# A plain first product, by token halves, in the first supertile of a fused attention and two-layer kernel

## The reference

```python
scores = matmul(q_c, k_c.T) / 8            # 576 chunks of 64 tokens, 64 dims (batch 8, heads 8, 9 chunks)
attn = exp(scores - max); attn /= sum(attn) + 1e-9
x = matmul(attn, v_c)                      # to [4608 tokens, 512]
h = x @ w_in;  g = max(h, 0) + alpha * min(h, 0);  y = g @ w_out      # 512 -> 2048 -> 512
h = y @ w_in2; g = h - tanh(h);                    out = g @ w_out2
```

## Time and profile before

| | us |
|---|---|
| median of 3 runs | 1644.78 (1644.63 to 1649.84) |
| the profiled execution | 1645.04 |
| its span, first to last instruction | 1643.2 |
| TensorE busy | 1584.7 (96% of the span) |
| VectorE, ScalarE, GpSimd busy | 977.2, 671.3, 328.6 |
| first product of supertile 0 begins | 41.28 |
| first product of supertile 1 begins | 206.87 |

### The profile page before, as it was taken

How to read it: one execution, slowest core, us unless ns; L and a number is a source line. 1 busy time by engine, 2 the same in 40 slices (tenths; PEclk the granted TensorE clock), 3 DMA queues, 4 the chain that set the end, 5 groups by cost and what they waited for, 6 DMA issues and landing times.

```text
span 1643.2 us, 26691 instructions
## 1 busy us (share of the span) xinstructions
PE 1584.7 (96%) x10512; PEld 1487.1 (90%) x10512; DVE 977.2 (59%) x1351; ACT 671.3 (41%) x995; POOL 328.6 (20%) x454
## 2 busy tenths in 40 slices
PE   4879999999999999999999999999999999999999
PEld 3878899989999999999989988988988988988987
DVE  5557868766785776676674562562662562562542
ACT  4566535535553554554553241242232232232221
POOL 3684556676564200000000000000000000000000
PEclk9999999999999999999999999999999999999999
DMA  5477688769879756755734843853853843843842
GB/s 206 170 280 251 232 311 339 263 238 363 277 251 333 285 181 215 269 175 183 298 140 152 311 178 129 330 181 127 334 180 124 334 178 125 335 175 127 295 178 76
DMA packets 72938, 375.04 MB, mean 228 GB/s; under 512 B 9072, under 2 KB 13168, under 8 KB 38256
## 3 DMA queue, kind: packets, MB, share of 16 engines
q1 hardware_dynamic: 63216, 341.87, 57.7%
q0 software_dynamic: 9600, 31.46, 5.2%
HBM read 308.29 MB, written 65.01 MB: 227 GB/s over the span
## 4 chain that ended last, share of the span: by engine, by line
PE 86%; DVE 4%; DMA 3%; POOL 3%; issue 2%; ACT 2%; SPq 0%; ACTq 0%; POOLq 0%; DVEq 0%
PE banks L522 13%; PE banks L523 13%; PE banks L524 13%; PE banks L551 7%; PE banks L553 7%; PE banks L552 7%; PE banks L585 5%; PE banks L586 5%; PE banks L584 5%; PE a_bank L584 3%; PE a_bank L585 3%; PE a_bank L586 3%; DMA raw<-in_weights 2%; POOL ring L339 1%; DVE go_lo L960 1%
## 5 line engine op out<-in xcount | busy, mean ns | idle before, releaser
L522 PE MATMUL banks<-xo_hi,ring 128*128 128x384 f32 x1344 | 453.4, 337 | 20.1 <-POOL ring L339 7.6
L524 PE MATMUL banks<-xo_hi,ring 128*128 128x384 f32 x1344 | 452.2, 336 | 0.0
L523 PE MATMUL banks<-xo_lo,ring 128*128 128x384 f32 x1344 | 452.1, 336 | 0.0
L960 DVE TENSOR_TENSOR go_lo<-g_full,go_hi 128x768 fp32r<-128x768 f32 x288 | 287.1, 999 | 252.1 <-ACT go_hi L746 251.4
L746 ACT CAST go_hi<-g_full 128x768 fp32r<-128x768 f32 x288 | 239.6, 837 | 366.3 <-PE banks L586 223.5
L551 PE MATMUL banks<-go_hi,ring 128*128 128x384 f32 x768 | 265.6, 346 | 13.9 <-DVE go_lo L960 8.7
L522 PEld LDWEIGHTS banks<-xo_hi,ring 128*128 128x128 f32 x1344 | 254.6, 189 | 24.7 <-POOL ring L339 14.4
L553 PE MATMUL banks<-go_hi,ring 128*128 128x384 f32 x768 | 257.0, 335 | 0.0
L552 PE MATMUL banks<-go_lo,ring 128*128 128x384 f32 x768 | 256.8, 334 | 0.0
L523 PEld LDWEIGHTS banks<-xo_lo,ring 128*128 128x128 f32 x1344 | 254.6, 189 | 0.4
L524 PEld LDWEIGHTS banks<-xo_hi,ring 128*128 128x128 f32 x1344 | 254.5, 189 | 0.0
(11 more groups left out here) (98 smaller groups left out, 1924.1 us busy)
## 6 DMA issues: line engine op xcount, KB each, us to landing
ring<-w_split SPq DMA_DIRECT2D x242, 1024.0 KB, 5.5
qkv<-in_chunks SPq DMA_DIRECT2D x60, 384.0 KB, 5.0
w_split<-ring SPq DMA_DIRECT2D x22, 1024.0 KB, 5.1
w_split<-made_first POOLq DMA_DIRECT2D x44, 256.0 KB, 5.8
w_split<-sums POOLq DMA_DIRECT2D x44, 256.0 KB, 5.6
y_between<-stage SPq DMA_DIRECT2D x12, 768.0 KB, 7.2
x_raw<-y_between SPq DMA_DIRECT2D x6, 1536.0 KB, 9.4
out<-x_raw SPq DMA_DIRECT2D x36, 256.0 KB, 6.6
```

The lines of the kernel that those rows point to most:

```text
L522: nc.tensor.matmul(h, hi, xo_hi[:, o, k, :], start=fresh and k == 0, stop=False, skip_group_check=not fresh)
L523: nc.tensor.matmul(h, hi, xo_lo[:, o, k, :], start=False, stop=False, skip_group_check=not fresh)
L524: last = nc.tensor.matmul(h, lo, xo_hi[:, o, k, :], start=False, stop=k == 1, skip_group_check=not fresh)
L960: nc.vector.tensor_tensor(go_lo[:, slot, :, :], g_of(n), go_hi[:, slot, :, :], ALU.subtract).then_inc(glo_ready, 1)
```

## The change

Only stage 0 changes in what it computes; the other stages find the same blocks in `w_dram`.

- Phase A of stage 0 becomes a plain product with 8 blocks a pair in place of 7: the first 32 token-half t = 0 with all of the weights (`first_product(0, m)`, m = 0 to 15, two blocks each), then t = 1 with the same 32 blocks. Four operands of the input are split (B11, B21, B12, B22), no sums.
- The 32 blocks are made as before (cast, low part), stored one by one (`store_block`, 256 KB), those of A21 to a new `w_a21`, and loaded again for the second half (`load_blocks`, groups 8 to 15).
- `first_product(0, 0)` to `(0, 4)` lie between the attention units 3 to 5 of supertile 0, whose `probs` get two more buffers.
- ScalarE reads each bank with two Relus (`act_first`), VectorE finishes it (`activate_first`).
- GpSimd makes the 32 sum blocks (S1 to S4 of 8 pairs), which stage 1 on need, with `keep_block`: 8 of them after the last of the 32 low parts, the other 24 each after one low part of the second product's blocks. It reloads raw weights for that into one buffer, `raw[:, 0]` (`load_again`); the raw weights of the second product share `raw[:, 1]`.
- Stage 0 has 96 blocks (`FIRST_BLOCKS`); block 64 + n is that of unit n. SP's `load_unit` calls stand after `store_block` of units 0, 1, 15, 19, 23 and 28.

```diff
+FIRST_BLOCKS, SLICES = 96, 32
+FIRST_GROUPS = FIRST_BLOCKS // PER_GROUP
...
+            def load_again(p):
+
+                for i in range(2):
+                    nc.gpsimd.dma_start(raw[:, 0, i, :], weights[p + PAIRS * i, :, 0:DM]).then_inc(raw_again_in, 16)
...
+            def keep_sum(layer, p, i, step, k):
...
+                if i:
+                    pool.wait_ge(made_step, step)
+                    pool.wait_ge(made_low, k)
+                if i == 0:
+                    nc.gpsimd.tensor_tensor(s3, a11, a21, ALU.subtract).then_inc(made_step, 1)
+                elif i == 1:
+                    nc.gpsimd.tensor_tensor(a21, a21, a22, ALU.add).then_inc(made_step, 1)
+                elif i == 2:
+                    nc.gpsimd.tensor_tensor(s2, a21, a11, ALU.subtract).then_inc(made_step, 1)
+                else:
+                    nc.gpsimd.tensor_tensor(s2, a12, s2, ALU.subtract).then_inc(made_step, 1)
+                pool.wait_ge(made_step, step + 1)
+                keep_block(layer, product_at(layer, (7, 5, 6, 3)[i], p), k, (s3, a21, s2, s2)[i])
+
+            def sum_of_first(k):
+
+                p, i = divmod(k, 4)
+                if i == 0:
+                    pool.wait_ge(raw_again_in, 32 * (p + 1))
+                keep_sum(0, p, i, k, k)
+                if i == 3 and p + 1 < PAIRS:
+                    pool.wait_ge(made_low, k + 1)
+                    load_again(p + 1)
...
-            for j in range(BLOCKS):
-                what, i, p = block_use(0, j)
-                if what == "product" and i == (6 if p else 1):
-                    weight_sums(0, j, p)
-                low_part(0, j)
-            pool.wait_ge(wlo_ready, BLOCKS)
+            for j in range(SLICES):
+                low_part(j)
+            pool.wait_ge(wlo_ready, SLICES)
+            load_again(0)
+            for k in range(8):
+                sum_of_first(k)
+            for n in range(units_in(0)):
+                low_part(2 * SLICES + n)
+                if n < 24:
+                    sum_of_first(8 + n)
...
+            def first_product(t, m):
...
+                for half in range(2):
+                    j = SLICES * t + 2 * m + half
+                    o = (B12, B22)[half] if t else (B11, B21)[half]
+                    weights_ready(0, j)
+                    if m == 0:
+                        pe.wait_ge(xlo_ready, x_count(0, o))
+                    w = block_of(0, j)
+                    for k in range(2):
+                        hi, lo = w[:, 0, k * P:(k + 1) * P], w[:, 1, k * P:(k + 1) * P]
+                        nc.tensor.matmul(h, hi, xo_hi[:, o, k, :], start=half == 0 and k == 0, stop=False)
+                        nc.tensor.matmul(h, hi, xo_lo[:, o, k, :], start=False, stop=False)
+                        last = nc.tensor.matmul(h, lo, xo_hi[:, o, k, :], start=False, stop=half == 1 and k == 1)
+                    last.then_inc(block_done, 1)
...
+            scores(5)
+            first_product(0, 0)
+            output(3)
+            first_product(0, 1)
+            transpose_attn(4)
+            first_product(0, 2)
+            output(4)
+            first_product(0, 3)
+            transpose_attn(5)
+            first_product(0, 4)
+            output(5)
+            for m in range(5, 16):
+                first_product(0, m)
+            for m in range(16):
+                first_product(1, m)
+            phase_b(0)
...
+            def act_first(t, m):
...
+                nc.scalar.activation(g_full[:, p, 2 * half + t, :], h, ACT.Relu)
+                nc.scalar.activation(part[:, m % 4, :], h, ACT.Relu, scale=-1.0).then_inc(h_read, 1)
...
+            for m in range(4, 16):
+                high_parts(2 * m + AHEAD)
+                act_first(0, m)
+            for m in range(16):
+                high_parts(SLICES + 2 * m + AHEAD)
+                act_first(1, m)
...
+                nc.vector.scalar_tensor_tensor(mine, part[:, m % 4, :], minus_alpha[:, f:f + 1], mine,
+                                               ALU.mult, ALU.add).then_inc(g_ready, 1)
...
+            def first_supertile():
+                for j in range(SLICES):
+                    if j >= 3 and j % 4 == 3 and j // 4 + 2 < PAIRS:
+                        load_raw(j // 4 + 2)
+                    store_block(j)
+                load_raw_second(0)
+                load_raw_second(1)
+                for group in range(8, 16):
+                    load_blocks(group)
+                for n in range(units_in(0)):
+                    if n % 2 == 1 and n // 2 + 2 < 16:
+                        load_raw_second(n // 2 + 2)
+                    store_block(2 * SLICES + n)
+                    if n in (0, 1, 15, 19, 23, 28):
+                        load_unit(UPS + (0, 1, 15, 19, 23, 28).index(n))
+                store_y(0, 0)
+                for group in range(FIRST_GROUPS, FIRST_GROUPS + RING - 1):
+                    load_group(group)
```

More of the change, by code:

```diff
@@ L77, in units_in, with unit_at @@
     return 32 if layer == 0 else 16
[L80 to L82 removed]
+def unit_at(s, n):
+    if s == 0:
+        return 2 * SLICES + n
+    if layer_of(s) == 0:
         return 55 if n == 0 else 56 + n
@@ L89, in unit_slice, with pairs_by @@
     return n % 16 // 2 + PAIRS * (n % 2)
[L92 to L116, removed]
+def pairs_by(q):
+    return sum(1 for p in range(PAIRS) if min(product_at(0, i, p) for i in range(1, 8)) < PER_GROUP * (q + 1))
 def fused_kernel(nc, chunks, weights, alpha, out):
@@ L318, in _, with low_part @@
         def _(pool):
[L319 to L339, removed]
+            def low_part(j):
+                here = block_of(0, j)
+                pool.wait_ge(whi_ready, split_index(j) + 1)
+                nc.gpsimd.tensor_tensor(here[:, 1, :], raw_of(j), here[:, 0, :], ALU.subtract).then_inc(wlo_ready, 1)
+            def load_again(p):
+                for i in range(2):
+                    nc.gpsimd.dma_start(raw[:, 0, i, :], weights[p + PAIRS * i, :, 0:DM]).then_inc(raw_again_in, 16)
             def load_raw2(c):
@@ L616, in phase_b @@
             def phase_b(s):
-                if layer_of(s) == 0:
+                if s == 0:
+                    second_product(s, 0)
+                    for n in range(1, units_in(0)):
+                        attention(s, n)
+                        second_product(s, n)
+                elif layer_of(s) == 0:
                     second_product(s, 0, (0,))
@@ L647, in _ @@
         def _(act):
-            made = {s: 0 for s in range(RUNS) if made_here(s)}
-            def high_part(s, j):
-                layer = layer_of(s)
-                what, i, p = block_use(layer, j)
-                if j % PER_GROUP == 0 and s * GROUPS + j // PER_GROUP >= RING:
-                    before, last = group_last(s, j)
-                    act.wait_ge(block_done, done(before, last))
-                    if made_here(before):
-                        act.wait_ge(w_stored[(s * GROUPS + j // PER_GROUP) % RING], 16 * stores_of(before, last))
-                if what == "product" and i in (3, 5, 6, 7):
-                    act.wait_ge(w_sum, 4 * (layer * PAIRS + p) + {7: 1, 5: 2, 6: 3, 3: 4}[i])
-                else:
-                    c = raw_chunk(layer, j)
-                    act.wait_ge(raw_in[c % 2], 32 * raw_loads(layer, c))
-                nc.scalar.copy(block_of(s, j)[:, 0, :], raw_of(layer, j)).then_inc(whi_ready, 1)
@@ L1052, in _ @@
             shift(0)
-            for u in range(UPS):
-                if u + 1 < UPS:
-                    shift(u + 1)
-                normalize(u)
+            shift(1)
+            normalize(0)
+            shift(2)
+            normalize(1)
+            shift(3)
+            normalize(2)
+            shift(4)
+            normalize(3)
             low_x(0, B11)
@@ L1192, in _ @@
             for i in range(RING):
-                sp.wait_ge(w_stored[i], 16 * sum(1 for g in range(i, GROUPS * RUNS, RING) if made_here(g // GROUPS)))
+                sp.wait_ge(w_stored[i], 16 * stores_of(FIRST_GROUPS - RING + i))
 def kernel(q, k, v, moe_w_in, moe_w_out, moe_alpha, moe2_w_in, moe2_w_out):
```

467 lines of the change are left out of this document (270 added, 197 removed).

## The result

The changed kernel takes 1722.81 us (median of 4, 1720.43 to 1724.37); its ratio to the kernel before, run beside it (median 1645.99 of 4), is 1.0462, 95% interval 1.0439 to 1.0484. The forecast was 1721 in a range of 1690 to 1754. The profiled execution has a span of 1720.9 us, 77.7 more than before.

What follows compares the result with a forecast made beforehand. GpSimd was taken to bound the opening supertile: unit 23's low part at 240 plus 43 gives 283 against 206.9, 76 us lost on about 1645. Forecast 1721 us, range 1690 to 1754.

Steps and rivals of the forecast that it cites:

- The bound: Stage 0, second phase: GpSimd's low parts, queued behind its sums, decide when the second product can go on.
- First product: Opening of stage 0: begins near 36, first_product 5 near 55, other 27 calls at 2.08 us end near 111.
- TensorE still waits in the first product, for raw DMA: Rival, first product: the change does not do what it says; moves little, since GpSimd sets the end; no separate chance.
- Last low part: GpSimd, first half: the last of 32 low parts at 69 us (64 to 73).
- The ninth sum: GpSimd behind 69: three reload gaps (21.9) and 8 sums x 3.7 (29.6) put it at 120.5 (101 to 132).
- The cadence: GpSimd, second phase: four units take 21.45 us (18.5 to 26.8), from sums, low parts and a reload gap.
- T: End of unit 23's low part on GpSimd in the second phase: 240 us (204.5 to 281).
- T + 43: End of supertile 0, with attention loads in SP's queue holding TensorE at units 9, 14, 17, 21.
- T + 24: End of supertile 0 without the hold by attention loads: 1702 us; rival's chance 0.2, including quick sums with the hold.
- Behind it both programs are the same on TensorE: Behind the first product of supertile 1 (206.87 before): same distance to the end as before.
- GpSimd keeps up: Rival, loop over n: sum and low part fit TensorE's 2.6 us a unit; 1634 us; chance 0.04.
- The heavy case: Second phase: every GpSimd step behind a go_lo difference slow from port sharing, four units nearer 26.8 us, time near 1748.

Runs made afterwards that it cites:

- e_tworaw: Changed kernel with a second buffer for GpSimd's reload of raw weights for the sums, first pair loaded ahead of low part 24: 1697.57 us.
- e_both: Changed kernel with attention loads 8 to 11 behind stores of units 11, 15, 19, 23 and ScalarE casting 3 blocks ahead, not 10: 1718.72 us.
- e_free: e_both with the loads of attention units 8 to 11 moved to behind the stores of units 7, 11, 15, 20: 1702.86 us.
- e_behind: Changed kernel with the last 24 of the 32 weight sums made behind all low parts of the second product: 1698.04 us.
- e_best: Changed kernel with VectorE's old order, ScalarE casting 3 ahead, earlier attention loads, two reload buffers and GpSimd's sums spread: 1656.98 us, ratio to before 1.0057.

## Why the prediction was right, and where that was luck

**The bound.** GpSimd's low parts behind its sums set the end of stage 0. Right; shown by e_tworaw, which touched GpSimd alone in stage 0.

**First product.** Its end was put at 111 and is at 111.5. But two errors cancel: first_product(0, 5) began at 44.1, not 55 (the start at 29.6 and not 36, no long slow phase), and the 27 calls behind it took 2.50 us each, not 2.08, with 8.1 us of waits (5.2 of them for ScalarE's Relu, which stood behind casts that waited 3.7 and 3.0 us for raw chunks) and a granted clock of 0.93 from 36 to 60 us. Its rival "TensorE still waits in the first product, for raw DMA" came true in this form, and moved little, as it said. Last low part: 67.0 for 69.

**The ninth sum**: 115.1 for 120.5. Eight sums took 3.4 us each, with store waits of 2.8 and 0.35 us only, and not 3.7; the three gaps, from the end of the step before the load's issue, took 6.7, 8.2 and 5.7 us, for 7.3.

**The cadence**: 21.0 us for four units against 21.45. Gaps ran from 4.3 (ahead of 134.00) to 7.5 us (ahead of 219.90) around the 6.1 taken. DMA moved 159 to 211 GB/s in the four windows, not 145. T: 230.7 for 240, most of it from the ninth sum.

**Who holds TensorE behind T** is the step that failed: "T + 43" from SP's queue alone, with "T + 24" if that hold did not exist. It came to T + 50, and removing the hold alone gave T + 52. The signs named for it failed too: no wait for L339's low parts (here L344), and 7.4 us of waits for attention loads in all. What the prediction left out is ScalarE: it was said to have room in the first product, by the sum of its durations, and got no term in the second, while its list stands 10 blocks ahead at a raw buffer that GpSimd frees. It hides SP's queue, and SP's queue hides it; only without both does stage 1 follow at T + 28. The size was not bad: with ScalarE out of the way the hold cost 17 us of stage 1's start, 11 of them behind T (e_both against e_free), where the prediction had 19. The 9 us by which T came early and the 7 us by which the rest came late cancel too, so that 1721 is within 2 us of the measured time is luck; that it lies in the range is owed to GpSimd's cadence.

**Not seen**: low_g(2) ahead of activate_c11, 0.68 us in each of six stages, 4.1 us. "Behind it both programs are the same on TensorE" was true of TensorE's list, not of whom it waits for.

**Rivals.** "GpSimd keeps up" would have needed 2.6 us for a sum and a low part; the quickest sum was 2.9.

Contention: GpSimd's two-input operations take 0.72 to 0.76 us or up to 1.6, and the timelines show when. From 110 to 231 us after there are 71 of them. 21 overlap in time a VectorE operation with both inputs in SBUF, and 10 of these took 0.91 to 1.47 us; the 50 others all took 0.72 to 0.75. Before, from 60 to 200 us, 36 of 92 overlap one, 25 of them took 0.90 to 1.56 us, and none of the 56 others more than 0.76. Two meetings, one begun by VectorE and one by GpSimd (a go_lo difference that meets nothing takes 0.95 us):

```profile
197.04 0.95 DVE L1085 TENSOR_TENSOR go_lo<-g_full,go_hi 128x768 fp32r<-128x768 f32 x1
...
197.20 1.38 POOL L364 TENSOR_TENSOR made_first<-sums,made_first 128x256 fp32r<-128x256 f32 x1
...
221.18 0.74 POOL L364 TENSOR_TENSOR made_first<-sums,made_first 128x256 fp32r<-128x256 f32 x1
...
221.29 1.44 DVE L1085 TENSOR_TENSOR go_lo<-g_full,go_hi 128x768 fp32r<-128x768 f32 x1
```

This agrees with what the Trainium skill says in "SBUF — State Buffer", section "SBUF: two separate sides", of taking turns for a whole instruction. The heavy case did not come because few steps met: VectorE was busy 2.5 and 11.6 of 30 us in the first two windows. All 24 low parts were quick (mean 0.74 us, against 0.91 before), but the 12 differences of kept blocks in made_first had a mean of 1.00.

On the loads, the prediction set the 2.6 and 5.7 us of the earlier trace rows beside the rule for loads; those are GpSimd's stores, and its loads had 3.4 and 6.2. That the fixed 2.0 us plus bytes of the Trainium skill, "DMA: Bandwidth & Descriptors", section "Anatomy of one DMA", an estimate of 2.6 us, would be the landing did not hold: the minimum of GpSimd's reloads was 3.4 and their median 5.1 us.

**Left open.** How much of e_behind's 25 us is due to the queues and how much to the order was not separated, nor how much of e_best's gain is due to spreading the sums. Whether a split in which ScalarE makes the sums' high parts would bring this first product below the kernel before was not tried; e_best misses by 0.6%, about 9.5 us.

## What to carry to other kernels

- Work put "beside" a stage must fit in the time until its result is read, on the engine that does it: here 64 low parts of 0.74 us and 32 sums of 3 us and more, with a reload exposed every fourth, before stage 1 could read them. Putting it behind the low parts moved the wait into the next stage; spreading it, with the other causes undone, made the loss small but left no gain.
- An engine that runs a fixed number of steps ahead is safe only while its own supplier is ahead of the consumer. When the supplier becomes the bound, the look-ahead turns into a block in front of the engine's other work. Look at what is queued behind each wait, not at the engine's busy share.
- Two queues that each hold the same engine hide each other: undoing one shows nothing. Before a cause is dismissed on such a result, look in that run's trace at what is waited for instead.

## What the runs showed of the hardware

A GpSimd operation on two 128x256 operands took 0.72 to 0.76 us alone; only where it overlapped a VectorE operation with both inputs in SBUF did it take more: in 10 of 21 such overlaps after (up to 1.47 us, from 110 to 231 us), in 25 of 36 before (up to 1.56, from 60 to 200 us). The go_lo difference of VectorE took 0.95 us, and 1.44 where GpSimd had begun first. TensorE's granted clock averaged 0.66 to 0.81 in the four windows in which it was busy 6 to 19 of 30 us. Behind the waits of 21.4, 6.5 and 13.7 us the matmuls stepped by 0.32 us (1.2 GHz) for 3.7, 2.7 and 2.7 us, in place of 0.17 us (2.4 GHz), so a stalled second phase pays a second time when it goes on.
